# Routing comparisons on broadcast tensors and 1 MB chunk loads, together with MoE transposes by DMA and VectorE and the down product two tiles behind

## What is computed

```python
def _attn_ref(q, k, v):                      # (4, 8, 768, 64)
    gamma = 1.0 - 2.0 ** (-5.0 - np.arange(H))
    for t in range(S):
        state = gamma * state + einsum('bhd,bhe->bhde', k[:, :, t], v[:, :, t])
        y[:, :, t] = scale * einsum('bhd,bhde->bhe', q[:, :, t], state)

def _moe_ref(x, w_gate, w_output_gate, w1, w2):   # x (3072, 512), 8 experts, inner 1024
    logits = x @ w_gate
    e_idx = np.argmax(logits, axis=1)
    gate_w = softmax(logits)[np.arange(N), e_idx]
    eom = sigmoid(x @ w_output_gate)
    for e in range(E):
        mask = e_idx == e
        h = np.maximum(x[mask] @ w1[e], 0.0)
        out[mask] = gate_w[mask, None] * eom[mask, e, None] * (h @ w2[e])

def _moe2_ref(x, w_in, w_out):               # inner 2048
    h = x @ w_in
    return (h - np.tanh(h)) @ w_out
```

## Time and profile before

| | |
|---|---|
| Three runs, median | 1138.88 us (1138.87 to 1140.42) |
| Profiled execution | 1138.32 us, its span 1136.5 us |
| TensorE busy | 1087.8 us, 96% of the span |
| VectorE busy | 665.3 us, 59% |
| ScalarE busy | 329.1 us, 29% |
| GpSimd busy | 360.9 us, 32% |
| Moved by DMA | 107.25 MB, mean 94 GB/s |

### The profile page before, as it was taken

How to read it: one execution, slowest core, us unless ns; L and a number is a source line. 1 busy time by engine, 2 the same in 40 slices (tenths; PEclk the granted TensorE clock), 3 DMA queues, 4 the chain that set the end, 5 groups by cost and what they waited for, 6 DMA issues and landing times.

```text
span 1136.5 us, 18848 instructions
## 1 busy us (share of the span) xinstructions
PE 1087.8 (96%) x5953; PEld 907.2 (80%) x5954; DVE 665.3 (59%) x1175; ACT 329.1 (29%) x632; POOL 360.9 (32%) x316
## 2 busy tenths in 40 slices
PE   8978797999999999999978999999999999999998
PEld 7867686888888888888766887888888888888887
DVE  4888975212212222222159787877876887777775
ACT  2432321222222222222112333333333333333333
POOL 2454549193663874874094000000000000000000
PEclk9998998999999999999988999999999999999999
DMA  9975645152433443443140001000000000100101
GB/s 338 340 253 193 226 147 159 63 175 90 155 115 120 148 156 114 154 146 122 37 130 10 19 10 46 9 18 37 18 18 37 18 18 0 55 0 0 38 1 37
DMA packets 44223, 107.25 MB, mean 94 GB/s; under 512 B 5280, under 2 KB 5664, under 8 KB 44192
## 3 DMA queue, kind: packets, MB, share of 16 engines
q1 hardware_dynamic: 31280, 77.73, 19.9%
q10 hardware_dynamic: 9072, 16.52, 4.6%
q0 software_dynamic: 3840, 12.59, 3.4%
HBM read 84.01 MB, written 22.81 MB: 94 GB/s over the span
## 4 chain that ended last, share of the span: by engine, by line
PE 82%; DVE 11%; issue 3%; DMA 2%; ACT 1%; POOL 0%; SPq 0%; DVEq 0%; ACTq 0%; POOLq 0%
PE banks L1025 17%; PE banks L1027 17%; PE banks L1026 17%; PE banks L1126 7%; PE banks L1128 7%; PE banks L1127 7%; PE banks L1058 2%; DVE onehot L646 2%; PE banks L1032 1%; PE banks L945 1%; PE banks L933 1%; PE banks L926 1%; DVE q_scaled L668 1%; DVE probs L675 1%; PE banks L1105 1%
## 5 line engine op out<-in xcount | busy, mean ns | idle before, releaser
L383 POOL TENSOR_TENSOR w_sb<-raw,w_sb 128x1024 fp32r<-128x1024 f32 x80 | 192.5, 2407 | 6.7
L1126 PE MATMUL banks<-x2T_hi,w_sb 128*128 (+1 forms) x384 | 154.3, 402 | 7.2 <-DVE g_sb L868 7.2
L1128 PE MATMUL banks<-x2T_lo,w_sb 128*128 (+1 forms) x384 | 152.0, 396 | 0.0
L1127 PE MATMUL banks<-x2T_hi,w_sb 128*128 (+1 forms) x384 | 151.7, 395 | 0.0
L1025 PE MATMUL banks<-w_sb,g_lo 128*128 128x512 f32 x384 | 149.8, 390 | 0.0
L1026 PE MATMUL banks<-w_sb,g_hi 128*128 128x512 f32 x384 | 149.7, 390 | 0.0
L1027 PE MATMUL banks<-w_sb,g_hi 128*128 128x512 f32 x384 | 149.6, 390 | 0.0
L396 POOL DMA_INDIRECT gathered<-y_sorted,row_back x20 | 22.1, 1107 | 364.3 <-DVE x_sb L833 363.7
L760 DVE TENSOR_TENSOR xsT_lo<-banks,xsT_hi 128x512 fp32r<-128x512 f32 x32 | 22.1, 691 | 159.1 <-ACT xsT_hi L521 159.1
L577 ACT ACTIVATE square<-banks 128x512 f32<-128x512 f32 x96 | 57.4, 598 | 196.0 <-PE banks L1128 196.0
L584 ACT ACTIVATE g_hi<-g_sb 128x512 fp32r<-128x512 f32 x96 | 60.7, 632 | 169.5 <-PE banks L1027 151.6
(11 more groups left out here) (137 smaller groups left out, 1914.4 us busy)
## 6 DMA issues: line engine op xcount, KB each, us to landing
raw<-in_weights SPq DMA_DIRECT2D x80, 512.0 KB, 3.4
xs_sb<-x_sorted ACTq DMA_DIRECT2D x32, 256.0 KB, 2.9
y_sorted<-ys_sb ACTq DMA_DIRECT2D x31, 256.0 KB, 2.1
kT_sb<-in_kT SPq DMA_DIRECT2D x24, 256.0 KB, 3.4
qT_sb<-in_qT SPq DMA_DIRECT2D x24, 256.0 KB, 4.1
kn_sb<-in_kn SPq DMA_DIRECT2D x24, 256.0 KB, 4.2
vn_sb<-in_vn SPq DMA_DIRECT2D x24, 256.0 KB, 4.8
out_rows<-out_sb SPq DMA_DIRECT2D x24, 256.0 KB, 2.2
```

The costliest lines, as they stand in the source:

```text
L383: nc.gpsimd.tensor_tensor(w_sb[:, s, 1, lo:hi], raw[:, p % RAW_SLOTS], w_sb[:, s, 0, lo:hi].bitcast(fp32), ALU.subtract).then_inc(piece_do ...
L1126: T.matmul(out_, w_lo, hi, start=first, stop=False)
L1127: T.matmul(out_, w_hi, hi, start=False, stop=False)
L1128: return T.matmul(out_, w_hi, lo, start=False, stop=last)
```

## The change

It consists of five parts.

1. **Routing.** `choose_expert` compares with `tensor_tensor` on a broadcast of the one column, where it used an instruction with a pointer to that column (`scalar_tensor_tensor`, `tensor_scalar`). One instruction becomes two, so there are seven links in the chain and not six.
2. **Loads of attention.** The four inputs of a chunk lie side by side in one array and come in one transfer of 1 MB (the first chunk in two of 512 KB). Of the six decay tables for the queries only the first is loaded; GpSimd makes the five others from it (`make_q_decay`). All tables, and the zeroing of the heads in `x_sorted`, are issued from ScalarE's queue.
3. **Transposes of the MoE.** The rows are loaded by four transfers, each a quarter of the columns into a quarter of the partitions, so that a transpose within blocks of 32 x 32 on VectorE completes them. `hid` is stored to memory (`hid_rows`), loaded back in another order (`hid_quads`) and transposed by VectorE in two halves. The host lays the weights out to match. `xsT` and `hidT` lie in SBUF, so `_hi` and `_lo` are made from there.
4. **Order.** `rows_out` runs two tiles behind: step i of TensorE is `hidden(i)` and `rows_out(i - 2)`. `hidT_hi` and `hidT_lo` have two buffers, and the loops hold two steps.
5. **Weights.** GpSimd splits the up weights of the next set once the last `hidden` of the old one is done, and only the down weights wait for `ys_done`. Half of the tenth set is split ahead of the gathers.

VectorE in the attention loop, from the largest logit of a chunk to its row: before,

The diff, cut to its core:

```diff
-                for dst, src in ((kT_sb, kT), (qT_sb, qT), (kn_sb, kn), (vn_sb, vn)):
-                    sp.dma_start(dst[:, c % RING], tile_of(src, b * CHUNKS + c)).then_inc(in_ready[c % RING], 16)
+                sp.dma_start(in_sb[:, c % RING].rearrange("p n d -> p (n d)"), tile_of(rows_in, b * CHUNKS + c))\
+                  .then_inc(in_ready[c % RING], 32)
...
+            for half in range(2):
+                cols = slice(half * 2 * D, (half + 1) * 2 * D)
+                sp.dma_start(in_sb[:, 0].rearrange("p n d -> p (n d)")[:, cols], rows_in[0][:, cols]).then_inc(in_ready[0], 16)
...
+            def split_pieces(m, s, before=None):
+                if before is not None:
+                    pool.wait_ge(hid_done, before * 2)
+                for p in range(W2_AT // PIECE):
+                    split_piece(m, s, p)
+                if before is not None:
+                    pool.wait_ge(ys_done, before)
+                for p in range(W2_AT // PIECE, SET_PIECES):
                     split_piece(m, s, p)
...
+            def make_q_decay(c):
+                nc.gpsimd.tensor_tensor(q_decay_sb[:, c].rearrange("p (a t) -> p a t", a=PAIRS),
+                                        q_decay_sb[:, 0].rearrange("p (a t) -> p a t", a=PAIRS),
+                                        q_step_sb[:, c].unsqueeze(2).to_broadcast([P, PAIRS, P]),
+                                        ALU.mult).then_inc(q_decay_made, 1)
             pool.wait_ge(k_decay_ready, 16)
-            for t in range(RING):
-                scale_keys(t)
+            scale_keys(0)
+            pool.wait_ge(q_decay_ready, 32)
+            make_q_decay(1)
+            scale_keys(1)
+            make_q_decay(2)
+            make_q_decay(3)
+            scale_keys(2)
+            make_q_decay(4)
+            make_q_decay(5)
             pool.wait_ge(heads_zeroed, 16)
...
-            pool.wait_ge(ys_done, before)
-            split_pieces(EXPERTS // 2, 0)
+            split_pieces(EXPERTS // 2, 0, before)
+            pool.wait_ge(hid_done, 2 * MOE_TILES)
+            for p in range(W2_AT // PIECE):
+                split_piece(EXPERTS // 2, 1, p)
...
+            act.dma_start(k_decay_sb[:], k_decay).then_inc(k_decay_ready, 16)
+            act.dma_start(decay_mask_sb[:], decay_mask).then_inc(mask_ready, 16)
+            act.dma_start(q_decay_sb[:, 0], q_decay).then_inc(q_decay_ready, 16)
+            act.dma_start(q_step_sb[:], q_step).then_inc(q_decay_ready, 16)
...
+            act.wait_ge(zeros_made, 2)
+            act.dma_start(x_sorted.rearrange("(e r) d -> r e d", e=EXPERTS)[0:P],
+                          zeros[:].unsqueeze(1).to_broadcast([P, EXPERTS, D])).then_inc(heads_zeroed, 16)
...
+                    act.wait_ge(xsT_done, i)
+                    row = act.value_load(load_row[0:1, bass.ds(i, 1)], min_val=0, max_val=EXPERTS * REGION_ROWS - P)
+                rows = x_sorted[bass.ds(row, P)].rearrange("(g b) c -> b g c", g=QUADS)
+                for quad in range(QUADS):
+                    cols = slice(quad * (D // QUADS), (quad + 1) * (D // QUADS))
+                    act.dma_start(xs_sb[quad * QUAD:(quad + 1) * QUAD], rows[:, :, cols]).then_inc(xs_ready, 16)
...
+            def store_hidden(i):
+                act.wait_ge(relu_done, i * 2 + 2)
+                act.dma_start(hid_rows.rearrange("i p f -> p i f"), hid[:].rearrange("p (i f) -> p i f", i=QUADS))\
+                   .then_inc(hid_stored, 16)
+            def load_hidden(i):
+                act.wait_ge(hid_stored, i * 16 + 16)
+                act.dma_start(hid_quads[:].rearrange("p g f -> p (g f)"), hid_rows.rearrange("i (b g) f -> (i b) (g f)", g=QUADS))\
+                   .then_inc(hid_ready, 16)
+            def hid_hi(i, number):
+                if number >= 2:
+                    act.wait_ge(ys_done, i - 1)
                 for n in range(2):
...
+            def moe_step(i, number):
+                relu(i, 0)
+                if number >= 1:
+                    hid_hi(i - 1, number - 1)
+                if number >= 3:
+                    store_rows(i - 3)
+                relu(i, 1)
+                store_hidden(i)
+                if number + 1 < MOE_TILES:
+                    x_hi(i + 1)
+                load_hidden(i)
+                if number + 2 < MOE_TILES:
+                    load_rows(i + 2)
...
-                V.scalar_tensor_tensor(out=ranked[:, 0], in0=router, scalar=top[:, bass.ds(t, 1)], in1=first_rank,
-                                       op0=ALU.is_equal, op1=ALU.mult).then_inc(route_chain, 1)
+                V.tensor_tensor(ranked[:, 1], router, top[:, bass.ds(t, 1)].to_broadcast([P, EXPERTS]), ALU.is_equal)\
+                 .then_inc(route_chain, 1)
                 dve.wait_ge(route_chain, t * ROUTE_LINKS + 2)
+                V.tensor_tensor(ranked[:, 0], ranked[:, 1], first_rank, ALU.mult).then_inc(route_chain, 1)
...
-                V.tensor_scalar(one(onehot, t), ranked[:, 0], route[:, 0:1], None, ALU.is_equal).then_inc(onehot_done, 1)
+                dve.wait_ge(route_chain, t * ROUTE_LINKS + 4)
+                V.tensor_tensor(one(onehot, t), ranked[:, 0], route[:, 0:1].to_broadcast([P, EXPERTS]), ALU.is_equal)\
+                 .then_inc(onehot_done, 1)
...
+                    dve.wait_ge(xsT_lo_done, i)
+                V.transpose(xsT[:].rearrange("p k (g b) -> p g k b", g=QUADS),
+                            xs_sb[:].rearrange("p g (k a) -> p g k a", k=DK)).then_inc(xsT_done, 1)
...
+            def transpose_hidden(i):
+                dve.wait_ge(hid_ready, i * 16 + 16)
+                dve.wait_ge(hidT_lo_done, i * 2)
+                for n in range(2):
+                    ks = slice(n * DK, (n + 1) * DK)
+                    V.transpose(hidT[:, ks].rearrange("p k (b g) -> p g k b", g=QUADS),
+                                hid_quads[:].rearrange("p g (k a) -> p g k a", k=FK)[:, :, ks]).then_inc(hidT_done, 1)
...
+            def moe_step(i, number):
+                if number >= 3:
+                    if number >= 4:
+                        dve.wait_ge(ys_stored, i * 16 - 48)
+                    copy_rows(i - 3)
+                if number >= 1:
+                    transpose_hidden(i - 1)
+                if number + 1 < MOE_TILES:
+                    transpose_rows(i + 1)
+                if number >= 1:
+                    hid_lo(i - 1, (number - 1) % 2)
+                if number + 1 < MOE_TILES:
+                    x_lo(i + 1)
...
-            def transpose_rows(i):
-                pe.wait_ge(xs_ready, i * 16 + 16)
-                for k in range(DK):
-                    last = T.transpose(at(0)[:, k * P:(k + 1) * P], xs_sb[:, k * P:(k + 1) * P], ident[:])
-                last.then_inc(xsT_done, 1)
...
+                if not first:
+                    pe.wait_ge(relu_done, i * 2)
...
+            def rows_out(i, number, par):
                 pieces = pe.value_load(w1_pieces[0:1, bass.ds(i, 1)], min_val=1, max_val=SETS * SET_PIECES)
                 slot = pe.value_load(w_slot[0:1, bass.ds(i, 1)], min_val=0, max_val=1)
                 pe.wait_ge(piece_done, pieces + (SET_PIECES - W2_AT // PIECE))
+                if number >= 3:
+                    pe.wait_ge(ys_copied, i)
                 pe.wait_ge(hidT_lo_done, i * 2 + 2)
...
             stay_warm(WARM_TAIL[2], still)
-            transpose_rows(0)
             stay_warm(WARM_TAIL[3], still)
             hidden(0, first=True)
             pe.wait_ge(tables_done, 1)
-            transpose_rows(1)
-            transpose_hidden(0)
             hidden(1)
-            transpose_rows(2)
-            rows_out(0)
-            transpose_hidden(1)
-            with pe.Fori(2, MOE_TILES) as i:
+            def moe_step(i, number):
                 hidden(i)
-                transpose_rows(i + 1)
-                pe.wait_ge(ys_copied, i - 1)
-                rows_out(i - 1)
-                transpose_hidden(i)
-            pe.wait_ge(ys_copied, MOE_TILES - 1)
-            rows_out(MOE_TILES - 1)
+                rows_out(i - 2, number, number % 2)
+            for i in range(2, 5):
+                moe_step(i, i)
+            with pe.Fori(5, MOE_TILES - 2, 2) as i:
+                moe_step(i, 5)
+                moe_step(i + 1, 6)
+            for i in (MOE_TILES - 2, MOE_TILES - 1, MOE_TILES):
+                if i < MOE_TILES:
+                    hidden(i)
+                rows_out(i - 2, i, i % 2)
+            rows_out(MOE_TILES - 1, MOE_TILES + 1, (MOE_TILES - 1) % 2)
```

180 lines of the change are left out of this document (84 added, 96 removed).

## The result

The changed kernel takes 1130.72 us (median of 10 runs, 1125.45 to 1135.37), the kernel before in the same series 1138.88 (1136.53 to 1140.42): ratio 0.9925, 95% interval 0.9908 to 0.9942. The profiled execution took 1131.54 us with a span of 1129.8. So the kernel is 0.75% faster, where 4.5% was forecast. Its ten runs lie in two groups, four from 1125.45 to 1126.70 and six, the profiled one among them, from 1129.89 to 1135.37; what parts them isn't shown.

A forecast was written before the change was run, and what follows sets the result against it. It took VectorE waiting for GpSimd to bound attention after its early chunks, and TensorE the MoE and last stage. 1136.5 - 20 + 1 - 26.6 (MoE) - 5 = 1085.9, plus 2.4 from span to median: 1088 us; 8-in-10 range 1072 to 1110.

The forecast's parts named there:

- Attention, -20: Attention routing: new comparisons are free beside GpSimd's scatter, 15 chunks take 82.5 us instead of 102.4, so -20 us.
- bound "0": Attention: the no-gain end of the -20 us term, 15 chunks staying at 6.83 us each.
- rival A: Attention: new comparisons meet key scaling and splits as often as before, gain under 10 us, 1098 to 1108 us; chance 0.20.
- Loads, +1: Attention loads: fewer bytes, but first chunks compete with the zeroing; 3 us gained to 4 lost, taken as +1 us.
- MoE steady, -33.3: MoE tiles: transposes leave TensorE, new work is covered, step 12.29 to 11.1 us over 28 steps, -33.3 us.
- Rival C: MoE: ring of store, load, transposes, rounding, relu sets the step, 10.7 us, 12.2 under weight loads; 1119 us; chance 0.12.
- The fear that splits hold up `xsT_lo`: MoE: `xsT_lo` may be held by a split, ready at 7.9 to about 11 of 11.1 us; cover just suffices.
- Entry +1.6: MoE entry: first load in four issues, +1.2, and transpose with its copies, about +0.4; +1.6 us.
- +2.2: MoE entry, second up product: transpose and ScalarE copy before `xsT_lo`, +1.4, and a possible hold, +0.8; +2.2 us.
- first step -4.5: MoE, step 1: it no longer has a down product, -4.5 us.
- The end, +7.4: MoE end: last up product to first gather 31.2 us instead of 23.8, down product of tile 29 4.5 late; +7.4 us.
- Last stage, -5: Last stage, first steps: four of eight weight splits lie before the gathers, freeing second and third step; -5 us.

The follow-up runs named there:

- r_routing: The kernel before with the routing comparisons on broadcast tensors (part 1) alone: 1139.09 us, ratio 1.0009 to the kernel before.
- b_keysfirst: The kernel before, old comparisons kept, with the key scaling put ahead of the scatter: 1125.99 us, ratio 0.9883 to the kernel before.
- r_loads: The kernel before with the 1 MB chunk loads and decay tables made on GpSimd (part 2) alone: 1140.88 us, ratio 1.0018 to the kernel before.
- m_noraw: The changed kernel with MoE and last-stage weight loads cut from 1024 to 64 columns, splits whole: 1108.49 us, ratio 0.9744 to the kernel before.
- f_ring: The changed kernel with ScalarE's and VectorE's MoE steps reordered, tokens' split a step ahead in two buffers, end reordered: 1098.30 us, ratio 0.9641 to the kernel before.
- f_swap: The changed kernel with `hid_hi` behind second relu, store and `x_hi`, `x_lo` ahead of `hid_lo`, `hid_rows` in two halves: 1115.26 us, ratio 0.9789 to the kernel before.
- f_all2: Parts 3 to 5 with reordered MoE steps, key scaling ahead of scatter, first set's splits 256 columns wide, tile 1's tokens ahead of gate tables: 1068.33 us.
- m_nosplit: The changed kernel with weight splits of sets 1 to 9 cut from 1024 to 128 columns, loads whole: 1146.30 us, ratio 1.0069 to the kernel before.

## Why the prediction was wrong, by its own steps

The sum was 1085.9, the span is 1129.8, and the 44 us are placed.

1. **Attention, -20: measured about 0. This step failed, and by its reason.** "So against the scatter the new form is free" came from one row, 110.27, at the very start of the scatter; `onehot` stands 0.6 us into it. The row of the held `onehot`, 110.89, was put down to the scatter, though it ended with the split (112.62 and 112.59), as the text itself said. The first of the two, 89.59, ends with the key scaling. The cause stood in the rows: what holds is the instruction queued behind the scatter. In the trace of before `onehot` starts 0.28 us into the scatter at 29.11 and at 34.20, and lasts 1.86 us with a key scaling behind it, 0.23 with nothing behind it. r_routing shows no gain from the form, b_keysfirst 13 us from the order with the old form. Its bound "0" was in the sum, and rival A priced 10 to 20 us for it. All 20 were lost. The rule cited from the Trainium skill, SBUF — State Buffer, section "Who interferes with whom", is not contradicted: key scaling and split read SBUF, and the two-input `onehot` waited for them. That it did so though its own recorded start came first is more than the rule says. The prediction's "The trace agrees" rests on the row 110.27 alone, which started before the scatter and shows nothing of either rule. What the prediction drew from the rule, that a small instruction would be free because it starts beside the scatter, is contradicted.
2. **Loads, +1: +2** (r_loads, +0.2 to +4). Right in sign and order. Items 1 and 2 together are 20.9 us of the miss.
3. **MoE steady, -33.3: -16.1.** TensorE's part was right: where nothing waits a step is 10.88 us, under the 11.1 and just under its bound of 11.0. The cover failed, which was to hide store, load and transposes. Store and load were sized 3.0 and 3.5; they had medians of 3.7 and 4.0 and went to 6.1 and 5.8, the transpose was 1.10 us a half instead of 0.7. The step that failed is "their consumer is the down product of the step after, so nothing waits": it looked at who consumes `hidT`, not at what is queued behind `hid_hi` on ScalarE. Rival C had the loop, with 10.7 us around and 1.5 more under load. It came out at 11.72 a step on the mean and 14.96 at worst, so C was the right mechanism with a chance of 0.12, and its price of 12.2 a step was half a microsecond too high. What C lacked is VectorE's order, `hidT_lo` ahead of `xsT_lo`. Miss: 17.2 us. The fear that splits hold up `xsT_lo` had a point, but they don't do it alone: m_noraw keeps them and has no wait. The advice against VectorE stands in the Trainium skill, VectorE: DVE Perf Modes, section "Rules for kernel authors"; the estimate of 1.24 us for 512 elements, made from its bf16 figure, is above the 0.70 and the 1.10 us of this trace.
4. **Both ends.** Entry +1.6 (measured 1.8), +2.2 (1.0) and first step -4.5 (-2.8): close. The end, +7.4, is +13.7. The wait was in the right place, before the down product of tile 29, but it was 7.5 us and not 4.5, the hidden rows landing late, and the products behind it ran at the lower clock: 0.86 in that stretch, 1.00 in f_ring's, where no wait is over 1.5 us. Miss: 6.3.
5. **Last stage, -5: -6.1** in the trace, and -3.8 for the part alone. Right.

The sum of the misses: 20.9 + 0.2 - 1.2 + 1.7 + 17.2 + 6.3 - 1.1 = 44.0. Of the marks named ahead, the transposes near 0.7, store and load under 7, `onehot` at 0.2 and chunks at 5.0 to 5.6 all failed. The wait before the third up product, about 2, was 3.6. The tokens' transposes (0.70) and, but for the one at 83.89, the free first comparison held. The mark for failure, chunks still near 6.8, is what came: 101.95 / 15 = 6.80. A and C were priced as rivals of one another, each alone; A's upper end and C's mechanism came together, and their prices on one sum, 1088 + 20 + 31, would have been 1139.

## What to carry to other kernels

Where a small VectorE instruction is long and ends with a GpSimd instruction, look at what stands in GpSimd's queue behind the one running, and change that order or cut it in pieces; another form of the small instruction gained nothing here. When work leaves the busy engine for transfers, write down the loop that they close on each in-order queue: an instruction that waits for a transfer should not stand ahead of the one whose result starts the next transfer, nor the work on the old tile ahead of what TensorE waits for next. Then longer transfers cost little (f_swap) or nothing (f_ring, f_all2), at the same bytes in the MoE.

## What the runs showed of the hardware

- A two-input or one-column VectorE instruction of 8 elements that starts 0.28 us or more into GpSimd's scatter lasts 0.17 to 0.49 us if nothing follows the scatter at once, and mostly 1.4 to 3.0 if a key scaling or a split does, to the end of that instruction. One that starts within 0.16 us of the scatter's start isn't held in either case, and neither was one at 0.43 us (new form) or 0.28 us (old form) ahead of a split alone. Why it is held before that instruction's recorded start isn't shown. With splits cut to 256 columns `onehot` lasted 0.17 to 0.45 us beside them.
- A VectorE transpose in 32 x 32 blocks of 128 x 512 float32 takes 0.70 us, and 1.10 us with the outputs four elements apart.
- A 512 KB store of the hidden rows had a median of 2.96 us and its load back 3.32 beside weight loads cut to 64 columns (m_noraw), 3.7 and 4.0 beside whole ones in the changed kernel, 6.1 and 5.8 at most, and a store took 9.0 in m_nosplit. The Trainium skill, DMA: Bandwidth & Descriptors, section "Queues, rings and completion order", says that each DMA engine takes turns between its queues packet by packet. In tiles 2 to 30 of the changed kernel the weights' queue moved 29.89 MB in 8208 packets, ScalarE's 43.79 MB in 38832, so 3.6 KB against 1.1 KB a packet on the mean; by that rule, if its packets are those that the profile counts, an estimate is that ScalarE's queue gets about a quarter of the engines while weights are queued. The 9.0 us agree with its direction. Against the packets' size as the cause: the store runs in packets of 1 KB and the load back in packets of 4 KB, as large as those of the weights, and both grew by about 0.7 us on the median. Other packet sizes weren't tried.
- The lower clock followed TensorE's longer waits: the granted clock is 0.94 over m_nosplit's tiles, with seven waits of 3.2 to 4.4 us, and 0.99 in f_all2's, where nothing waits. In the changed kernel it came behind the waits of 3.0, 3.6, 3.9 and 7.5 us; in the tiles behind those of 0.4 to 1.6 us it stays 1.00.

Left open: the entry's last 5 us, and how much of the attention a split entirely on another engine would still give.
